# One rounding on ScalarE moved twelve instructions later in a fused attention and two-layer kernel

## The reference

```python
def _moe2_ref(x, w_in, conv_w, w_out) -> np.ndarray:
    B, S, D_ff = (*x.shape[:2], w_in.shape[1])
    h = np.maximum(x @ w_in, 0.0)
    ...
    for k in range(K):
        conv_out += conv_w[k][None, None, :] * hp[:, k:k + S, :]
    gate = 1.0 / (1.0 + np.exp(-conv_out))
    return (h * gate @ w_out).astype(np.float32)
```

## Time and profile before

| | us |
|---|---|
| median of 3 runs | 381.51 |
| lowest, highest | 379.96, 382.63 |
| profiled execution | 381.0 |
| its span, first to last instruction | 378.9 |
| PE busy | 372.1 |
| DVE busy | 279.4 |
| ACT busy | 220.1 |
| POOL busy | 169.1 |

### The profile page before, as it was taken

The page is one execution under the profiler, slowest core; times in us unless marked ns, Lnnn a source line. Parts: engine busy times, 40 slices in busy tenths (PEclk is TensorE's granted clock), DMA queues, the critical chain, the costliest instruction groups (busy, mean ns, idle before and its releaser), DMA issues.

```text
span 378.9 us, 6125 instructions
## 1 busy us (share of the span) xinstructions
PE 372.1 (98%) x2166; PEld 328.5 (87%) x2166; DVE 279.4 (74%) x639; ACT 220.1 (58%) x399; POOL 169.1 (45%) x137
## 2 busy tenths in 40 slices
PE   8999999999999999999999999999979999999996
PEld 4799999998888888898888889889768889999996
DVE  5676868665887899999888864347068886989782
ACT  3686868785776786443545173454186779945030
POOL 4999999997345200400000055000199626335720
PEclk9999999999999999999999999999999999999999
DMA  6999879516100353412131341000600000002123
GB/s 204 400 417 385 309 299 330 220 50 246 1 0 3 112 200 134 160 50 83 42 85 42 83 168 55 3 0 2 222 0 0 2 0 0 3 0 85 42 97 112
DMA packets 15760, 43.98 MB, mean 116 GB/s; under 512 B 4464, under 2 KB 5744, under 8 KB 15728
## 3 DMA queue, kind: packets, MB, share of 16 engines
q1 hardware_dynamic: 15728, 43.57, 32.1%
HBM read 32.16 MB, written 11.40 MB: 115 GB/s over the span
## 4 chain that ended last, share of the span: by engine, by line
PE 92%; DMA 4%; SPq 1%; DVE 1%; issue 1%; ACT 1%
PE bank L636 32%; PE bank L798 19%; PE bank L872 15%; PE bank L686 9%; PE bank L669 5%; PE bank L655 4%; PE bank L778 3%; DMA wo<-w_out_in 2%; DMA qk_sb<-qk_laid 2%; PE bank L697 1%; PE bank L811 1%; SPq L321 1%; DVE biased L1370 0%; ACT bank L1155 0%; ACT bop L1195 0%
## 5 line engine op out<-in xcount | busy, mean ns | idle before, releaser
L798 PE MATMUL bank<-b_ops,a_ops 128*128 128x512 f32 x324 | 75.5, 391 | 0.0
L798 PEld LDWEIGHTS bank<-b_ops,a_ops 128*128 128x128 f32 x324 | 60.5, 188 | 12.3
L636 PE MATMUL bank<-v_span,win 128*128 128x512 f32 x288 | 66.7, 391 | 2.2 <-ACT h_sb L1144 2.2
L636 PEld LDWEIGHTS bank<-v_span,win 128*128 128x128 f32 x288 | 53.7, 188 | 13.7 <-ACT h_sb L1144 2.6
L572 POOL TENSOR_TENSOR win<-winraw,win 128x1024 fp32r<-128x1024 f32 x4 | 9.6, 2404 | 69.7 <-ACT win L1078 69.7
L872 PE MATMUL bank<-bop,a_place 128*128 128x384 f32 x160 | 40.6, 334 | 0.0
L947 ACT ACTIVATE pT<-bank 128x512 f32<-128x512 f32 (+1 forms) x48 | 26.8, 558 | 18.5 <-PE bank L686 17.4
L636 PE MATMUL bank<-wth,xT 128*128 128x512 f32 x144 | 35.9, 399 | 0.0
L636 PE MATMUL bank<-uT,wch 128*128 128x384 f32 x192 | 34.8, 336 | 0.0
L636 PEld LDWEIGHTS bank<-uT,wch 128*128 128x128 f32 x192 | 33.8, 188 | 0.6
L686 PE MATMUL bank<-v_sb,pT 128*128 128x65 f32 x264 | 33.7, 269 | 0.0
(11 more groups left out here) (128 smaller groups left out, 745.0 us busy)
## 6 DMA issues: line engine op xcount, KB each, us to landing
qk_sb<-qk_laid SPq DMA_DIRECT2D x7, 792.0 KB, 10.1
w_raw<-w_tok_laid SPq DMA_DIRECT2D x6, 768.0 KB, 11.2
a_kept<-stage SPq DMA_DIRECT2D x6, 768.0 KB, 4.8
a_ops<-a_kept SPq DMA_DIRECT2D x6, 768.0 KB, 4.9
v_sb<-v_laid SPq DMA_DIRECT2D x5, 780.0 KB, 7.7
a_kept<-stage SPq DMA_DIRECT2D x9, 384.0 KB, 3.5
a_ops<-a_kept SPq DMA_DIRECT2D x9, 384.0 KB, 3.1
out<-acc SPq DMA_DIRECT2D x6, 384.0 KB, 2.4
```

The source lines that it names most:

```text
L636: last = pe.matmul(dst, w[a], m[b], start=(i == 0 and j == 0), stop=(i == n - 1 and j == 2))
L798: last = pe.matmul(y_bank(s)[:], a_ops[:, slot, hi, blk, :], b_ops[:, side, blk, lo, :], start=(blk == 0 and j == 0), stop=(blk == NT - 1 ...
```

## The change

One call in ScalarE's list moves: high_a(0) stood behind relu(7) and ahead of first_tap(2), the third unit's; now it stands behind first_tap(4), the fifth unit's, and ahead of relu(13). Nothing else differs: the same instruction with the same wait, and the lists of the other engines are the same.

```diff
@@ -1220,7 +1220,6 @@
             high_v(14)
             high_v(15)
             relu(7)
-            high_a(0)
             first_tap(2)
             high_b(0, 1)
             relu(8)
@@ -1233,6 +1232,7 @@
             relu(11)
             relu(12)
             first_tap(4)
+            high_a(0)
             relu(13)
             first_tap(5)
             sigmoid(4)
```

## The result

The changed kernel takes 378.31 us in the median of 7 runs (378.22 to 378.58), the kernel before 381.51 (379.96 to 382.65): ratio 0.9913, interval 0.9889 to 0.9936. That is 3.2 us, where 2.3 had been forecast. The profiled executions lie 2.6 us apart in time (381.0 and 378.37) and 2.3 us in span.

The account below looks back on a forecast made before the run. PE was taken to bound the kernel, so only removing its idle time helps: removed 2.33 us, added 0, moved 0, so 381.5 - 2.3 = 379.2 us; own range 378.3 to 380.2, with rivals and scatter 377.5 to 381.4.

Parts of the forecast that it names:

- The stall and its size: PE ahead of hidden(9), waiting for relu(8) held behind high_a(0)'s wait for wo: 2.33 us lost, start to start.
- relu(8) in time, and the next deadlines: ScalarE after the move: relu(8) ends 4.6 us before hidden(9) wants it; relu(9) to relu(12) each have over 4 us.
- The moved instruction at no price: high_a(0) behind first_tap(4): its 1.06 us lie where ScalarE would wait for PE, wo landed 5.3 us earlier; price nothing.
- The transfer beside a busy ScalarE and VectorE: The wo transfer now overlapping ScalarE and VectorE work: cost taken as 0; upper end, 22 us at w_theta's rate.
- this is the ceiling of what this edit can give: PE's stall ahead of hidden(9): 2.33 us is the most the edit can gain, since no later matmul waits.
- 381.5 - 2.3: Whole kernel: median before less the removed stall, nothing added or moved, giving 379.2 us, ratio 0.994.
- More than the ceiling: Rival: output stage has hidden waits and gains too from gates started 7 us earlier; 377.5 us or less, chance 0.03.
- theory A2: Experiments' theory: wo's landing time, differing between runs, explains the medians' extra 0.9 us and the 2.7 us scatter before.

Follow-up runs that it names:

- the experiment behind relu(8): The kernel before with high_a(0) moved to just behind relu(8), ahead of first_tap(3): 378.76 us, ratio 0.9915.
- The double transfer: The changed kernel with w_out loaded twice, one after the other, ScalarE and GpSimd waiting for the second: 378.39 us, ratio 0.9913.
- second profile: The kernel before, unchanged, profiled once more to pair a landing time of wo with a span: 382.55 us.
- half the fillers: The kernel before with 8 calls of unused identity matmuls on PE ahead of hidden(9), filling part of the stall: 381.02 us.
- the first experiment: The kernel before with high_a(0) one place later, behind first_tap(2) and ahead of high_b(0, 1) and relu(8): 380.12 us, ratio 0.9958.
- the stall in the changed kernel: The changed kernel with PE waiting ahead of hidden(9) for the first of GpSimd's four sums: 380.26 us, ratio 0.9962.

## Why the prediction was right, and its one wrong term

**The stall and its size.** Right. PE's loss was put at 2.33 us, start to start and not the 2.18 of the bracket. The spans differ by 2.3, and the output stage starts at 315.22 for a forecast of 315.3. That the forecast for one profile also fits the runs has some luck in it: the stall of before is not the same in every run (see below), and the profiled one is near the mean of the held ones.

**relu(8) in time, and the next deadlines.** Right to 0.2 us each: relu(8) at 269.18 (forecast 269.0), relu(9) ends at 272.50 (272.4), relu(10) starts at 274.80 (274.7, the forecast end less its 0.39), relu(12) ends at 277.94 (277.9). The margin of relu(10) in before, of hundredths, came back in the experiment behind relu(8), where PE lost some 0.3 us around it.

**The moved instruction at no price.** Right: it ran at 278.66 (forecast 278.8) without a wait, and ScalarE then waited for PE. The double transfer moved the landing to 282.4, short of the 283.8 from which cost was reckoned, and cost nothing. But that run also shows the path behind the landing longer than reckoned: from 282.4 to the end of relu(14) at 287.2 it is 4.8 us, where the prediction had some 4.2. By this row the cost would begin at a landing of about 283.3, which is an estimate; it was not tried.

**The transfer beside a busy ScalarE and VectorE.** Taken as 0, with 22 us as the upper end. The landing took 9.5 us after the issue, beside 7 us of work of each, and PE did not slow down. The stretch of the changed kernel that answers to the first of the earlier trace rows:

```profile
263.38:274.46 11.08, 11.08 (x51) 9.17 (x50) 7.23 (x9) 7.03 (x11) 0.63 (x1) 1.00 0.57 191
```

Before it was 9.29, but the kernel before also showed 9.36 in its second profile and 9.51 in the one with half the fillers, so 9.5 is in its own scatter. The rule of the Trainium skill (SBUF — State Buffer, Who interferes with whom) that a DMA and a computing engine do not slow each other has here the row that was missing, and it agrees.

**The wrong term.** The step that failed is "this is the ceiling of what this edit can give", and with it the sum "381.5 - 2.3". It priced the stall as idle time alone, from one profile in which the clock held; behind it stands the prediction's first premise, that a change can bring time only where it removes idle time of PE. In 24 of 58 runs the stall also brought the clock down. The means show the two terms: before 381.50 over all 58 runs, 380.65 over the 34 with the clock held, and the changed kernel 378.37. The held runs are 2.28 us above the changed kernel, where the forecast term was 2.33. The fallen ones are 2.05 us above the held, which over all runs is 24/58 x 2.05 = 0.85. Together that is 3.13 us between the means. The medians of the seven runs differ by 3.2; a median of two groups depends on how many runs fall into each, and over all 58 runs of before it is 381.23, which makes 2.9.

Of the 2.05 the profile shows 1.6 as lost clock. The rest fits longer stalls in the fallen runs, by an estimate from the spans. The changed kernel's span is 376.3 to 376.6. Taking 376.5 from the spans of the held runs of before, 377.9 to 379.5, leaves stalls of 1.4 to 3.0 us, 2.2 in the mean. Taking off 1.6 of lost clock as well, those of the fallen runs, with spans of 380.5 to 381.2, had 2.4 to 3.1 us, 2.7 in the mean. This rests on one profile for the 1.6, so it is likely and not shown.

"More than the ceiling" was a rival, with chance 0.03, but for the wrong reason: it looked for hidden waits in the output stage. There are none.

**What was readable beforehand.** The scatter of 2.7 us in three runs was quoted and put aside as noise. In a PE-bound kernel with one stall it was worth asking whether the stall, or what it costs, is the same in every run.

**The remaining scatter.** Kernels that wait for wo on PE's path reach over 1.3 to 1.7 us with the clock held (before, the first experiment, the stall in the changed kernel, the fillers); those in which PE never waits for it, over 0.4 to 0.6. Three profiles in which hidden(9) waits for relu(8) in the order of before have landings of 9.29, 9.36 and 9.51 us after the issue, and hidden(9) starts 2.33, 2.41 and 2.56 us late. So, as far as these profiles show, a later landing goes into the time one for one where PE waits for it, and not where PE doesn't, which is what is left of theory A2.

## What to carry to other kernels

An engine that works in order hands on a wait to all that stands behind it, so an instruction that waits for a transfer and whose result is wanted much later belongs behind those that others want at once; here PE wanted relu(8) within 5 us, and the output stage wanted the rounding 40 us later. Price a stall of PE from start to start of its matmuls, and then ask about its clock: one profile may show only one of the two prices. Where the runs of a kernel fall into groups, compare their mean clocks before taking the scatter for noise.

## What the runs showed of the hardware

The granted clock fell behind a single gap of PE of 2.25 us, in a stretch otherwise busy, and not always: by their mean clocks and times it did so in 24 of 58 runs of the same program. With an idle time of 1.4 us (12 runs) and 1.7 us (12 runs) in the profiles it never fell, with 3.2 us it fell in all 6 and with 10.7 us in all 4. In the profile with 2.25 us idle it fell only 0.5 us after PE was at work again; with 3.2 and 10.7 us it fell within the idle time. In these three profiles, with 2.25, 3.2 and 10.7 us idle, the clock was low for 3.4, 6.8 and 10.2 us, and the matmuls behind the gap lost 1.6, 2.7 and 2.0 us.

The first profile of before had 2.18 us idle and no fall, and by the estimate from the spans some held runs had stalls of up to 3.0 us, so the length of the gap alone does not decide in between. It seems to matter all the same: by that estimate 16 of the 34 held runs of before had stalls of 2.0 us or less and none of the fallen ones did. What else decides was not tried.

A transfer of 2048 KB alone on the queue landed 8.6 to 9.5 us after its issue, from one execution to the next; a repeat of it straight behind the first took 8.4 and 8.7.
